# Attention in steps of four heads: the transposes of a set go behind the weighing of the set before

## The reference, cut to what matters

```python
scores = scale * np.matmul(q, k.transpose(0, 1, 3, 2))
keep = is_global | is_local
scores = np.where(keep, scores + bias, -1000000000.0)
a = np.exp(scores - np.max(scores, axis=-1, keepdims=True))
a = a / (np.sum(a, axis=-1, keepdims=True) + 1e-09)
attn = np.matmul(a, v)
...
h = x @ w_in
x = (h * (1.0 / (1.0 + np.exp(-h)))) @ w_out
...
for e in range(E):
    out += P[:, e:e + 1] * (np.maximum(x @ w1[e], 0.0) @ w2[e])
```

## Time and profile before

| | |
|---|---|
| median of 3 runs | 1411.77 us (1410.89 to 1414.84) |
| the profiled execution's own time | 1412.56 us |
| its span, first to last instruction | 1410.8 us |
| TensorE busy | 1377.9 us, 98% |
| VectorE busy | 799.8 us, 57% |
| ScalarE busy | 621.2 us, 44% |
| GpSimd busy | 310.9 us, 22% |
| mean granted TensorE clock | 0.992 |

### The profile page before, as it was taken

One profiled execution on the slowest core, in us unless ns is written; L12 is line 12 of the kernel. 1 busy time (PEld: TensorE's weight loads), 2 busy tenths in 40 slices (PEclk: granted clock), 3 DMA queues, 4 the chain that ended last, 5 costly groups with the idle time before them and its releaser, 6 DMA issues.

```text
span 1410.8 us, 19905 instructions
## 1 busy us (share of the span) xinstructions
PE 1377.9 (98%) x7345; PEld 1257.8 (89%) x7345; DVE 799.8 (57%) x1459; ACT 621.2 (44%) x1319; POOL 310.9 (22%) x372
## 2 busy tenths in 40 slices
PE   7998999999999999999999999999999999999998
PEld 6877999999998889898998989898898989899897
DVE  6576757647728555464645546664644646464452
ACT  6675535425334344262534426363543526253350
POOL 5211404030303130302213030312303021230300
PEclk9999999999979999999999999999999999999999
DMA  8401312221212121212222121321212122121211
GB/s 211 105 18 33 98 51 62 65 84 46 75 31 69 52 90 46 75 48 88 75 61 90 45 76 46 127 82 56 89 37 90 46 78 81 59 86 42 75 31 60
DMA packets 64594, 97.88 MB, mean 69 GB/s; under 512 B 18416, under 2 KB 33776, under 8 KB 64496
## 3 DMA queue, kind: packets, MB, share of 16 engines
q1 hardware_dynamic: 63968, 96.31, 22.8%
q10 hardware_dynamic: 528, 0.26, 0.1%
HBM read 93.41 MB, written 3.15 MB: 68 GB/s over the span
## 4 chain that ended last, share of the span: by engine, by line
PE 86%; DVE 8%; ACT 2%; POOL 2%; DMA 1%; issue 1%; SPq 0%; ACTq 0%; DVEq 0%
PE bank L650 38%; PE bank L715 35%; PE bank L712 6%; PE bank L562 2%; DVE up_l L1210 2%; PE bank L526 1%; PE bank L539 1%; PE bank L734 1%; POOL up_raw L459 1%; DVE hid_l L1257 1%; DVE hid_h L1255 1%; DMA up_raw<-w_up 1%; DVE parts L1226 1%; ACT parts L944 1%; DVE xc_l L1233 1%
## 5 line engine op out<-in xcount | busy, mean ns | idle before, releaser
L650 PE MATMUL bank<-xc_h,up_h 128*128 128x384 f32 x1120 | 377.8, 337 | 6.6 <-ACT bank L933 3.5
L650 PE MATMUL bank<-xc_h,up_l 128*128 128x384 f32 x1120 | 375.8, 336 | 0.0
L650 PE MATMUL bank<-xc_l,up_h 128*128 128x384 f32 x1120 | 375.6, 335 | 0.0
L715 PE MATMUL bank<-down_h,hid_h 128*128 128x512 f32 x768 | 300.1, 391 | 1.9 <-DVE down_l L1215 1.9
L715 PE MATMUL bank<-down_l,hid_h 128*128 128x512 f32 x768 | 300.3, 391 | 0.0
L715 PE MATMUL bank<-down_h,hid_l 128*128 128x512 f32 x768 | 300.3, 391 | 0.0
L459 POOL TENSOR_TENSOR up_raw<-up_raw 128x256 f32<-128x256 f32 x80 | 77.8, 973 | 928.9 <-DMA up_raw<-w_up 928.9
L1210 DVE TENSOR_TENSOR up_l<-up_raw,up_h 128x512 fp32r<-128x512 f32 (+1 forms) x240 | 204.7, 886 | 66.6 <-ACT up_h L873 66.5
L650 PEld LDWEIGHTS bank<-xc_h,up_h 128*128 128x128 f32 x1120 | 211.0, 188 | 13.1 <-issue 5.5
L650 PEld LDWEIGHTS bank<-xc_l,up_h 128*128 128x128 f32 x1120 | 210.9, 188 | 3.1 <-issue 0.2
L650 PEld LDWEIGHTS bank<-xc_h,up_l 128*128 128x128 f32 x1120 | 210.8, 188 | 0.0
(11 more groups left out here) (113 smaller groups left out, 1527.9 us busy)
## 6 DMA issues: line engine op xcount, KB each, us to landing
up_raw<-w_up SPq DMA_DIRECT2D x80, 512.0 KB, 3.7
down_raw<-w_down SPq DMA_DIRECT2D x160, 256.0 KB, 2.8
q_sb<-qT SPq DMA_DIRECT2D x12, 256.0 KB, 4.0
v_sb<-v SPq DMA_DIRECT2D x24, 128.0 KB, 4.0
out<-x_sb SPq DMA_DIRECT2D x12, 256.0 KB, 2.6
k_sb<-kT SPq DMA_DIRECT2D x11, 256.0 KB, 4.3
k_sb<-kT ACTq DMA_DIRECT2D x1, 256.0 KB, 3.8
vg_sb<-v SPq DMA_DIRECT2D x16, 4.0 KB, 2.4
```

What stands on the lines that cost most here:

```text
L650: mm = nc.tensor.matmul(ps[:, 0:HALF], a[quad % UP_BUFS][:, w, k, :], b[x][:, k, :], start=(n == 0 and not add), stop=(n == 5), skip_group ...
L715: mm = nc.tensor.matmul(ps[:], x[a][:, t // 3, t % 3 * P:t % 3 * P + P], w[b], start=start, stop=stop)
```

## The change

The order within a step is rewritten on three engines. On TensorE the transposes of set g-1 go from behind the scores to behind the weighing of set g-2 (and behind the global weighing), ahead of the output transpose. On ScalarE and VectorE the copies go from the middle of step g+1 to the start of step g+2: ScalarE's behind the copy of `x_sb`, VectorE's as the first instruction of the step. No instruction is added or dropped, and no semaphore or buffer is changed.

```diff
--- before.py
+++ after.py
@@ -585,8 +585,6 @@
                             score(m)
                         if g in before_turn:
                             before_turn[g]()
-                        for pair in pairs(g - 1, rows):
-                            turn(pair)
                         row = row_due(g, 3, rows)
                         if row is not None and row % QB >= 2:
                             turn_global(row)
@@ -596,6 +594,8 @@
                             weigh(pair)
                         if row is not None and row % QB >= 2:
                             weigh_global(row)
+                        for pair in pairs(g - 1, rows):
+                            turn(pair)
                         row = row_due(g, 4, rows)
                         if row is not None:
                             turn_x(row)
@@ -826,6 +826,9 @@
                         row = row_due(g, 5, rows)
                         if row is not None:
                             copy_x(row)
+                        for pair in pairs(g - 2, rows):
+                            if pair % 2 == 1:
+                                copy_probT(pair)
                         for n, m in enumerate(heads(g, rows)):
                             if n == SET // 2:
                                 turned_away(g, rows)
@@ -836,9 +839,6 @@
                             between[g]()
 
                 def turned_away(g, rows):
-                    for pair in pairs(g - 1, rows):
-                        if pair % 2 == 1:
-                            copy_probT(pair)
                     row = row_due(g, 3, rows)
                     if row is not None and row % QB >= 2:
                         copy_gprob(row)
@@ -1124,6 +1124,9 @@
 
                 def attend(steps, rows, between={}):
                     for g in steps:
+                        for pair in pairs(g - 2, rows):
+                            if pair % 2 == 0:
+                                copy_probT(pair)
                         for n, m in enumerate(heads(g, rows)):
                             if n == SET // 2:
                                 turned_away(g, rows)
@@ -1140,9 +1143,6 @@
                     row = row_due(g, 4, rows)
                     if row is not None:
                         normalise(row)
-                    for pair in pairs(g - 1, rows):
-                        if pair % 2 == 0:
-                            copy_probT(pair)
 
                 def general_distances(b, qb):
                     before = [b * QB * MASK_STEPS + qb * MASK_STEPS]
```

## The result

The changed kernel takes 1416.03 us (median of 8 runs, 1414.47 to 1418.69), the kernel before 1413.49 in the runs taken with it (8, from 1410.89 to 1415.17). The ratio is 1.0027, with an interval of 1.0016 to 1.0039: slower, clear of the noise, by 0.16% to 0.39%. A second timing (run e8, beside the kernel before and e5 to e7) gave 1415.55 (12 runs) against 1412.99 (35 runs), ratio 1.0018, interval 1.0009 to 1.0028. So the change costs about 2.5 us by the medians.

A forecast was written before the change was run, and what follows sets the result against it. The prediction took TensorE, busy for 98% of the span, to bound the kernel. Its terms, 0 + 0 + 1.6 us on 1412.56, gave 1414.2, in terms of a median 1413.5 us, with a range of 1410.0 to 1417.0.

The forecast's parts named there:

- Steps 18 to 23, +1.6 us: End of the attention stage: weighing waits for VectorE's copy behind its subtractions, so the stage ends 1.6 us later.
- The walk: Steps 18 to 23 followed in the new order with old durations; stage ends near 112.1 us, not 110.55.
- The boundary on TensorE: Weighing instead of transposes behind the scores: taken as 0, with about 1 us kept to each side.
- may lose 0.1: Step 13, with its short scores: the global transpose's need of the copy of x may cost 0.1 us.
- Steps 3 to 17 otherwise dense: Steady steps: the 1.12 us of scores cover the copies, no gap on TensorE, 0 us.
- rival 2: Slower in every step: weighing waits for copies in steady steps too; total +6.6 us, 1418.4 us; chance 10%.
- About 0.3%, 4.2 us: Whole kernel: the smallest difference said to be measurable; within it 0.80, slower 0.15, faster 0.05.
- The sum: Whole kernel: 0 + 0 + 1.6 us on 1412.56 gives 1414.2; as a median 1413.5 us, +0.1%.
- What was given as a sign of error: Steady-step idle before weighing or length not 4.37 or 4.90; stage end before 110.5; clock under 1 between 17 and 120 us.
- Rival 1 (the clock): The 2.25 us gap in step 20 makes TensorE's clock fall: 1.7 us, total +3.3, 1415.1 us; chance 13%.
- Rival 3 (nothing to see): Late attention steps: gaps only change their names, 4.3 us of stalls before and after, 1411.8 us; chance 17%.
- rival 4 (faster): Weighing pays nothing behind the scores (-3.3 us) and stalls of steps 18 to 22 shrink: 1407.1 us; chance 6%.

The follow-up runs named there:

- e8: The change again, unaltered, timed beside the kernel before: 1415.55 us, ratio 1.0018.
- e5: Kernel before with the next stage's eight pieces placed one at the end of each of steps 16 to 23: 1412.89 us, ratio 0.9996.
- e7: As e5, with TensorE's second product of the next stage ahead of the global transpose in step 25: 1414.03 us, ratio 1.0007.
- e10: The change with GpSimd's fourth sum of x moved ahead of its packing of row 9: 1414.62 us, ratio 1.0020.
- e2: The change, but in steps 18 to 21 VectorE makes its copy ahead of its two subtractions: 1412.64 us, ratio 1.0001.
- e4: The change with all eight pieces of the next stage moved to the end of step 23: 1417.81 us, ratio 1.0032.
- e3: Kernel before with all eight pieces of the next stage moved to the end of step 23: 1412.09 us, ratio 0.9993.
- e1: The change's copies on ScalarE and VectorE, with TensorE's order as in the kernel before: 1416.47 us, ratio 1.0022.
- e9: Kernel before with GpSimd's fourth sum of x moved ahead of its packing of row 9: 1412.42 us, ratio 1.0000.
- e11: Kernel before with GpSimd's sum early, second product early, next-stage pieces one each in steps 20 to 22, five in 23: 1411.21 us, ratio 0.9991.
- e12: e2 with GpSimd's fourth sum early and the second product ahead of the global transpose: 1411.92 us, ratio 0.9999.

## Why the prediction was right and wrong

- **Steps 18 to 23, +1.6 us: right, in mechanism, place and size.** Measured +1.45 (e8: +1.44). The walk had step lengths of 6.3, 6.5, 6.1, 5.45 and 4.95 us for steps 19 to 23; measured were 6.34, 6.48, 6.03, 5.50 and 4.80. The waits were to be 1.25, 2.25, 1.3 and 1.2; the timeline shows 0.86, 2.03, 0.72 and 1.05 put down to the copy, and 0.28 in step 19 before the global transpose. These are 4.9 us where I had 6.0, but the profile lists a matmul beyond the start of the next, and so lists less idle time than is lost; over the 27.8 us of dense work the stage is 5.8 us longer. That the largest would be in step 20, through a subtraction that stays long beside GpSimd, is shown by e10; that it is the copy's place behind the subtractions, by e2.
- **The boundary on TensorE, "so I take 0": the step that failed.** It measured +0.65 us over steps 3 to 17, in six profiles with the new order (62.01 to 62.05) against six with the old (61.35 and 61.36), and 0.14 more over steps 18 to 23 where nothing else is in the way (27.83 in e4, 27.69 in e3). In e1, with the new copies and TensorE's old order, a plain step has its old 3.93 us; with the new order it has 3.98. It is the term that was mis-sized: the weighing pays 0.19 behind the scores where the transposes paid 0.15, 0.04 to 0.05 in a step, and 0.16 in step 13, where "may lose 0.1" stood. The row I leaned on, the transposes' own 0.15, is a price of other instructions than those that now stand there. The bounds of 1 us held it.
- **Steps 3 to 17 otherwise dense: right.** No weighing waits in a steady step. The cover is the 1.12 us of scores, as said; rival 2 (5 us) did not come.
- **"About 0.3%, 4.2 us, is what a measurement of this kernel can tell from no change": this step failed too.** No row is given for it. It is about the spread of the three runs of before (1410.89 to 1414.84), but what counts is how closely two medians can be told apart. Eight runs of each kernel gave an interval of 1.0016 to 1.0039, about 0.12% or 1.6 us to each side, so they tell 2.5 us from nothing, where I had put 0.80 on no change. The boundary alone would not have mended this: with it the sum, 2.1 us, still lies under 4.2.
- **The sum**: 0 + 0 + 1.6 should have been 0.65 + 1.45 = 2.1, and the medians say 2.5. The 0.4 between them is open; the gap before the first product behind the attention, 1.66 us in before, was 2.19 and 1.78 in the two profiles of the change. The time measured, 1416.03, is 2.5 over the forecast of 1413.5 and lies in the range, near its upper end. Of these 2.5 us, 1.7 are the base: the forecast stood on the median of three runs, 1411.77, and the eight runs of before gave 1413.49. That the range held them is owed to the room left for the rivals; the forecast's own range ended at 1415.5.
- **What was given as a sign of error** did appear in part: steps of 4.41 in place of 4.37. The rest of the signs of the forecast came: idle time before the weighing in steps 19 to 22, put down to VectorE's copy, about 2 us in step 20, the wait for the global probabilities gone, line 639 near 112.
- **Rival 1 (the clock)**: out, by e8: the 2.03 us of step 20 cost no clock in two profiles of the change, the 3.98 us of e4 did. The Trainium skill (TensorE: Matmul & The Clock Gate, Why this matters for your kernels) advises against long idle gaps between bursts of matmuls, since the clock goes back to its lower level in them. The runs agree at e4's gap; for the shorter gaps no length divides those that cost clock from those that did not (see the end). **Rival 3 (nothing to see)** and **rival 4 (faster)**: out, by both intervals.
- **What I overlooked**: that the transposes wait for the copies through their banks (e1). It would not have changed the forecast, since in the change the transposes stand behind the weighing, which waits for the same copies; it spoiled the expectation for e1.

## What to carry to other kernels

Where an engine's queue holds work of another stage, put the short copy that the busiest engine waits for ahead of it, not behind; the copy fits into the queue's own wait for its input, and moving it was worth 3.0 us of a 33.6 us stage here, though it brought the total only level with the kernel before (1.0001). Reordering dense work on the busiest engine is not free even at constant work: price each boundary by a row with the same two instructions, and if there is none, keep a range. A walk through the queues with durations and releases from one profile gave five step lengths to 0.15 us here; it holds as long as every wait in the code, bank reuse too, is in it.

## What the runs showed of the hardware that was not expected

- The runs of one kernel spread over 8 us (before: 1409.98 to 1418.47 in 35 runs), and most of that is TensorE's granted clock: from 0.988 to 0.994 in the same runs. A fit over those 35 gives 0.73 us of time for each us of clock lost. It hides gains and losses of 1 to 2 us, as in e7, e9 and e11. The longest fall lies outside the attention, in the same place in the profiles of before, the change, e3 and e8: 96 products of 128x8 (line 734, from 391.7 us on in before) run back to back, and between 390 and 425 us, with TensorE listed as busy for 34.5 of 35 us, the mean granted clock is 0.76 in before, 0.71 in the change and 0.80 in e8.
- Versions that shorten the attention (e7, e11, e12) had a lower mean clock than before (0.9903 to 0.9907 against 0.9914 to 0.9925). Whether the shorter attention causes it, or whether it is chance, is open; e1, which lengthens the attention, has 0.9907 as well. The length of the gap at the attention's end does not decide it alone: e11 has a fall of the clock behind a gap of 2.63 us there, and e12, with the same 2.63, has none, while e5 and e10 have falls behind 2.00 and 1.84 us, and the change, with 2.19, has none.
- A subtraction of 128x512 on VectorE took 0.69 us alone and 2.15 us when it began beside GpSimd's sum of 1.83 us. It ended 0.55 us behind the sum (88.93 + 1.83 and 89.16 + 2.15). In e2, where the copy made it begin 0.93 us into the sum, it took 1.44 us and again ended 0.55 us behind it. So the two hardly overlap.
